# Product with the values in unsplit fp32 on two column groups, one key tile a step, loops written out

## What is computed

```python
# attention: batch 2, 8 heads, 768 tokens, head size 64
q_bucket, k_bucket = ...                 # 6 sign bits of q @ proj and k @ proj
scores = scale * np.matmul(q, k.transpose(0, 1, 3, 2))
scores = np.where(q_bucket == k_bucket, scores, -1000000000.0)
attn = np.exp(scores - np.max(scores, axis=-1, keepdims=True))
attn = attn / (np.sum(attn, axis=-1, keepdims=True) + 1e-09)
x = np.matmul(attn, v)
# second layer: gate = sigmoid(causal convolution of x, 5 taps), d_model 512
y = gate * (x @ w_val) @ w_out
# third layer: mixes of y with its previous token, d_ff 1024
k = np.maximum(xk @ w_k, 0.0); v = k * k @ w_v
out = sigmoid(xr @ w_r) * v
```

## Time and profile before

| | |
|---|---|
| median of 3 runs | 560.13 us (557.92 to 560.45) |
| span of the profiled execution | 556.6 us |
| its start up to step 0 of the first pair | 22.3 us |
| pair 0, pair 6 (pairs 1 to 5 alike) | 30.5, 31.5 us |
| pair 7 up to the second chunk's convolution | 44.3 us |
| from there to the end | 270.8 us |
| PE busy | 504.8 us, 91% of the span |
| DVE, ACT, POOL busy | 384.0, 327.1, 279.0 us |
| granted TensorE clock, pairs 0 to 6 | 1.00 of 2.4 GHz |

### The profile page before, as it was taken

The page is one execution under the profiler, slowest core; times in us unless marked ns, Lnnn a source line. Parts: engine busy times, 40 slices in busy tenths (PEclk is TensorE's granted clock), DMA queues, the critical chain, the costliest instruction groups (busy, mean ns, idle before and its releaser), DMA issues.

```text
span 556.6 us, 12146 instructions
## 1 busy us (share of the span) xinstructions
PE 504.8 (91%) x3744; PEld 463.4 (83%) x3744; DVE 384.0 (69%) x732; ACT 327.1 (59%) x745; POOL 279.0 (50%) x314
## 2 busy tenths in 40 slices
PE   2699999999999999997895879899799799799997
PEld 0488888878788888875795879899799799799997
DVE  2488887879788787979989778357557638633421
ACT  2398898989899998996744443242251341334140
POOL 4075574747567575757244363462550652544340
PEclk9999999999999999999898989899899899899999
DMA  8958293865839384662100000100100100000101
GB/s 232 217 134 189 98 204 100 204 153 153 206 98 204 113 193 109 140 147 113 39 2 2 0 1 1 39 1 2 38 0 0 38 0 0 20 19 1 39 1 39
DMA packets 20796, 45.74 MB, mean 82 GB/s; under 512 B 3744, under 2 KB 8864, under 8 KB 20768
## 3 DMA queue, kind: packets, MB, share of 16 engines
q1 hardware_dynamic: 20768, 45.38, 32.3%
HBM read 17.06 MB, written 3.15 MB: 36 GB/s over the span
## 4 chain that ended last, share of the span: by engine, by line
PE 62%; DVE 24%; issue 5%; ACT 3%; SPq 2%; DMA 2%; DVEq 1%; POOL 1%; ACTq 0%
PE ps L729 23%; PE ps L690 12%; PE ps L700 12%; PE ps L713 10%; DVE gate L886 10%; DVE tmp_a L984 3%; DVE gate L883 2%; PE ps L669 2%; DVE tmp_b L982 2%; DMA k<-hot_k 2%; DVE tmp_b L987 2%; PE ps L718 2%; DVE pt_lo L863 1%; DVE negmax L855 1%; SPq L245 1%
## 5 line engine op out<-in xcount | busy, mean ns | idle before, releaser
L863 DVE TENSOR_TENSOR pt_lo<-ps,pt_hi 128x384 fp32r<-128x384 f32 x192 | 97.8, 550 | 22.3 <-ACT pt_hi L524 22.0
L855 DVE TENSOR_REDUCE negmax<-ps 128x1 f32<-128x768 f32 x96 | 91.3, 951 | 27.2 <-PE ps L690 27.2
L690 PE MATMUL ps<-k,q 128*128 128x384 f32 x384 | 92.6, 364 | 11.7 <-DMA k<-hot_k 9.2
L516 ACT ACTIVATE probs<-ps,negmax 128x768 f32<-128x768 f32 x96 | 86.2, 898 | 16.8 <-DVE negmax L855 16.2
L700 PE MATMUL ps<-ident,probs 128*128 128x128 f32 x576 | 86.4, 281 | 7.4 <-DVE pt_lo L863 6.7
L700 PEld LDWEIGHTS ps<-ident,probs 128*128 128x128 f32 x576 | 64.9, 141 | 28.7 <-DVE pt_lo L863 13.5
L524 ACT ACTIVATE pt_hi<-ps 128x384 fp32r<-128x384 f32 x192 | 83.9, 488 | 6.7 <-PE ps L700 6.0
L690 PEld LDWEIGHTS ps<-k,q 128*128 128x128 f32 x384 | 64.0, 193 | 25.3 <-issue 11.4
L713 PE MATMUL ps<-pt_hi,vv 128*128 128x256 f32 x288 | 82.2, 315 | 0.0
L713 PE MATMUL ps<-pt_lo,vv 128*128 128x256 f32 x288 | 72.7, 282 | 0.0
L886 DVE SCALAR_TENSOR_TENSOR gate<-x,conv_sb,gate 128x256 f32<-128x256 f32 x96 | 64.2, 668 | 8.3 <-DVE gate L883 0.2
(11 more groups left out here) (93 smaller groups left out, 1257.8 us busy)
## 6 DMA issues: line engine op xcount, KB each, us to landing
k<-k_hi SPq DMA_DIRECT2D x32, 192.0 KB, 3.0
q<-q_hi SPq DMA_DIRECT2D x32, 192.0 KB, 3.7
w_raw<-w SPq DMA_DIRECT2D x8, 640.0 KB, 5.2
raw_q<-qT SPq DMA_DIRECT2D x8, 384.0 KB, 3.0
raw_k<-kT SPq DMA_DIRECT2D x8, 384.0 KB, 3.6
raw_v<-v SPq DMA_DIRECT2D x16, 192.0 KB, 3.9
k<-k_lo SPq DMA_DIRECT2D x16, 192.0 KB, 4.0
q<-q_lo SPq DMA_DIRECT2D x16, 192.0 KB, 4.1
```

What stands on the lines that cost most here:

```text
L516: act.activation(probs[par][:, :], score[par], ACT.Exp, bias=negmax[:, t % TILES:t % TILES + 1], accum_out=sums[:, t % TILES:t % TILES + 1 ...
L690: last = pe.matmul(ps[:, 2 * par + half, 0:HALF], qq[h][:, q], kk[h][:, half * HALF:(half + 1) * HALF], start=first, stop=not first)
L855: dve.tensor_reduce(negmax[:, t % TILES:t % TILES + 1], score[t % 2], AX.XY, ALU.max, negate=True)\
L863: dve.tensor_tensor(pt_lo[g % 2][dst], tbank[u].rearrange("p (k q) -> p k q", q=P), pt_hi[g % 2][dst], ALU.subtract).then_inc(lo_done, 1)
```

## The change

- The product with the values no longer splits anything. `vals` holds the values as loaded, `pt` the transposed probabilities of a whole head, double buffered. ACT copies the first half of each transposed tile (`first_half_up`), DVE the second (`second_half_up`).
- `product(head, kts)`: for one key tile two fp32 matmuls with 64 x 384 out, on column groups 0 to 63 and 64 to 127, one for each half of the queries. Key tile n of the head before is taken in step n of a head (`PV_STEPS`). The last head's product comes as a block at the end.
- The reciprocals are made once a head; POOL widens them (`widen_reciprocals`), three transposes (`spread`, in the fifth step, tt = 4, through bank 4) lay them out like the product, ACT copies them (`reciprocals_up`), and DVE multiplies the product straight from PSUM into `x` (`normalise`). POOL's part in it, the splits of v, `o_parts` and ACT's copies of the product are gone.
- All of `project` is at t = 0, `match` at t = 3 to 6.
- `x` is one stretch of tokens with a halo only at its start; the copies of halos are gone, `save_last` is a plain copy.
- All loops are written out, waits are on constants. `s_v` has one more wait (`relu_done`), `place` waits in front of each DMA for both heads.

```diff
-        tbank = [ps[:, 4 + s, 0:3 * P] for s in range(2)]
-        o_ps = ps[:, 6, 0:GQ]
-        r_ps = ps[:, 6, GQ:2 * GQ]
+        tbank = [ps[:, 4 + s, 0:HALF] for s in range(2)]
+        tbank3 = [t.rearrange("p (k q) -> p k q", q=P) for t in tbank]
...
+R_STEP = 4
+PV_STEPS = {n: (n,) for n in range(KT)}
+
+MATCH_STEPS = (3, 4, 5, 6)
...
+            def spread(head):
...
+                pe.wait_ge(rcpw_done, head + 1)
+                pe.wait_ge(up_done[0], turn_r(head))
+                for j in range(3):
+                    last = pe.transpose(tbank[0][:, j * P:(j + 1) * P], rcp_w[:, j, :, :], ident[:, :])
+                last.then_inc(tr_done[0], 1)
+
+            def product(head, kts):
...
+                h = head % 2
+                if kts[0] == 0:
+                    pe.wait_ge(v_in[h], 16 * (head // 2 + 1))
+                    pe.wait_ge(up_done[0], turns0(head, KT - 1) + 1)
+                    pe.wait_ge(up_done[1], KT * (head + 1))
+                    wait(pe, x_done, 2 * head)
+                for kt in kts:
+                    for n in range(2):
+                        last = pe.matmul(ps[DH * n:DH * (n + 1), 6, 0:HALF], vals[h][:, kt, :],
+                                         pt[h][:, kt, n * HALF:(n + 1) * HALF],
+                                         start=kt == 0, stop=kt == KT - 1, tile_position=(0, DH * n))
+                if kts[-1] == KT - 1:
+                    last.then_inc(pv_done, 1)
...
+            for g in range(PAIRS * TILES):
+                i, t = divmod(g, TILES)
+                head, tt = divmod(g, KT)
+                if g + 2 < PAIRS * TILES:
+                    scores(g + 2)
+                transposes(g)
+                if tt == R_STEP and head:
+                    spread(head - 1)
+                if i < LAST:
+                    if t == 0:
+                        project(i + 1)
+                    if t in MATCH_STEPS:
+                        match(i + 1, MATCH_STEPS.index(t))
+                elif t >= TILES - 2:
+                    pe.wait_ge(xlo_done, 1)
+                    s_val_tile(0, 2 * (t % 2))
+                    s_val_tile(0, 2 * (t % 2) + 1)
+                if tt in PV_STEPS and head:
+                    product(head - 1, PV_STEPS[tt])
+            spread(NHEADS - 1)
+            product(NHEADS - 1, tuple(range(KT)))
...
+            def second_half_up(g):
+                head, tt = divmod(g, KT)
+                if tt == 0:
+                    wait(dve, pv_done, head - 1)
+                dve.wait_ge(tr_done[1], g + 1)
+                dve.tensor_copy(pt[head % 2][:, 3:6, tt * P:(tt + 1) * P], tbank3[1]).then_inc(up_done[1], 1)
...
+            def normalise(head):
+                rows = (LO, HI)[head % 2]
+                dve.wait_ge(pv_done, head + 1)
+                dve.wait_ge(up_done[0], turn_r(head) + 1)
+                for n, part in enumerate((LO, HI)):
+                    dve.tensor_tensor(x[rows, head // 2, HALO + n * HALF:HALO + (n + 1) * HALF],
+                                      ps[part, 6, 0:HALF], r_sb[part, :], ALU.mult).then_inc(x_done, 1)
...
+                if tt == 0 and head:
+                    add_eps(head - 1)
+                if g + 2 < PAIRS * TILES:
+                    tile_max(g + 2)
+                if tt == 0 and head:
+                    reciprocals(head - 1)
+                second_half_up(g)
+                if tt == 0 and head >= 2:
+                    normalise(head - 2)
...
-                dve.tensor_scalar(z[:, :, 0:1], z[:, :, GQ:GQ + 1], carry[:, bass.ds(c + 1, 1)], None, ALU.mult)\
-                    .then_inc(hist_done, 1)
+                if (c + 1) % CPB:
+                    dve.tensor_copy(z[:, :, 0:1], z[:, :, GQ:GQ + 1]).then_inc(hist_done, 1)
+                else:
+                    dve.memset(z[:, :, 0:1], 0.0).then_inc(hist_done, 1)
```

More of the change, by code:

```diff
@@ L47, with wait, turns0, turn_r @@
 W2_PIECE = W2 // W2_PIECES
[L50 to L56, removed]
+R_STEP = 4
+PV_STEPS = {n: (n,) for n in range(KT)}
+MATCH_STEPS = (3, 4, 5, 6)
+PLACED = 8 * 16
+def wait(eng, sem, count):
+    if count > 0:
+        eng.wait_ge(sem, count)
+def turns0(head, tt):
+    return KT * head + tt + max(0, head - 1) + (1 if head >= 1 and tt > R_STEP else 0)
+def turn_r(head):
+    if head == NHEADS - 1:
+        return turns0(NHEADS, 0)
+    return turns0(head + 1, R_STEP) + 1
 def build(nc, qT, kT, v, proj, w1, w2, conv, mu_k, mu_r, codes, out):
@@ L361, in normalise @@
-            def normalise(i, j, g):
-                h, n = divmod(g, GROUPS // 2)
-                rows = (LO, HI)[h]
-                pool.wait_ge(o_up, j * GROUPS + g + 1)
-                own(i)
-                settled()
-                part = [o_parts[rows, n % 2, k, :] for k in range(3)]
-                step(i, pool.tensor_tensor(part[0], part[0], part[1], ALU.add))
-                own(i)
-                step(i, pool.tensor_tensor(x[rows, j // 4 * CPB + n, j % 4, HALO:XW], part[0], part[2], ALU.mult))
-                own(i)
-                pool.sem_inc(x_done, 1)
@@ L447, in _ @@
-            pairs(pool, body)
+                               base=0, pattern=[[-1, P]], channel_multiplier=1).then_inc(ident_up, 1)
+            low_parts(0)
+            for i in range(PAIRS):
+                if i:
+                    widen_reciprocals(2 * i - 1)
+                if i < LAST:
+                    low_parts(i + 1)
+                split_w(i)
+                if i == LAST:
+                    x_low(0)
+                widen_reciprocals(2 * i)
+            widen_reciprocals(NHEADS - 1)
@@ L618, in s_r @@
             def s_r(c):
-                after(act, o_done, c, DT, 0)
+                wait(act, o_done, c * DT)
                 for m in range(DT):
@@ L636, in _ @@
             tanh_gate(1)
-            def chunk(c, nxt, pre):
+            for c in range(CHUNKS):
                 act.wait_ge(mixlo_done, (c + 1) * 2 * DT)
-                if nxt:
+                if c + 1 < CHUNKS:
                     s_val(c + 1)
-                    if isinstance(c, int) and c == 0:
+                    if c == 0:
                         w2_high((2, 3))
@@ L778, in _ @@
-            pairs(pe, body)
-            output(PAIRS - 1, GROUPS - 1, 0)
-            output(PAIRS - 1, GROUPS - 1, 1)
+            for g in range(PAIRS * TILES):
+                i, t = divmod(g, TILES)
+                head, tt = divmod(g, KT)
+                if g + 2 < PAIRS * TILES:
+                    scores(g + 2)
+                transposes(g)
+                if tt == R_STEP and head:
+                    spread(head - 1)
+                if i < LAST:
+                    if t == 0:
[8 more added lines that the diff above has]
+                    product(head - 1, PV_STEPS[tt])
@@ L831, in chunk @@
                 s_v(c)
-            chunks(pe, chunk)
         @block.vector
@@ L858, in low_parts @@
[L858 to L864 removed]
+                    wait(dve, placed[B], PLACED * p)
@@ L959, in gated @@
+            add_eps(NHEADS - 1)
+            dve.wait_ge(pv_done, NHEADS - 1)
+            reciprocals(NHEADS - 1)
+            normalise(NHEADS - 2)
             def gated(c, m):
```

642 lines of the change are left out of this document (230 added, 412 removed).

## The result

The changed kernel takes **574.62 us** (median of 4 runs, 572.84 to 578.94) against 559.80 (4 runs, 557.92 to 560.45): ratio 1.027 [1.022, 1.032]. The direction was forecast, the size was not: +1.2% had been forecast (567 us), +2.7% came. The profiled execution is the slowest of the four: 578.94 us with a span of 577.1.

A forecast was written before the change was run, and what follows sets the result against it. PE was taken to bound the pairs, DVE the end of attention. Terms 17.5 - 3.2 + 4.3 - 12.0 = +6.6 on the 556.6 span gave 563.2; with 3.5 around it, 567 us, range 546 to 590.

The forecast's parts named there:

- The new wait: First product matmul of heads 2 to 15 waits some 2 us for DVE's `normalise`, 14 times; step 4.62 us.
- the rival without the wait: DVE is ahead, so the wait for `x_done` isn't felt: -27, 540 us; chance 0.07.
- The excursion: PE's move into column groups for one key tile: 0.97 us, 0.70 data and 0.27 going in and out.
- the switch is hidden: Rival: going in and out of column mode costs nothing behind the transposes, -24, 543 us; chance 0.15.
- the groups don't overlap: Rival: column groups of 64 run one after the other, +0.69 on 96 key tiles, +66, 633 us; chance 0.04.
- The clock: Rival: granted clock falls after each new wait, 14 x 1.5 = +21, 588 us; chance 0.10.
- Pairs 1 to 6: Attention's middle pairs: 34.4 us each against 31.47, +2.9 a pair, +17.5 together.
- the two steps with `spread`: Fifth step of each head: three transposes 0.33 and about 0.35 waiting for ACT's copy, 0.68 more.
- The tail: Second chunk's taps to the end: three chunks -6.9, clock falls gone -4.5, halos outside -0.6, together -12.0.
- Pair 0: First pair: six steps without product 12.5 us, second six 14.8; 27.3 against 30.5, -3.2.
- Pair 7: Last pair and block, up to the second chunk's taps: 48.7 against 44.3 us, +4.3, bounds 0 and +9.
- The start: Stretch up to step 0 of pair 0: 22.3 us, no change forecast.

The follow-up runs named there:

- the kernel in threes: Changed kernel with normalise first, spread behind the product, high parts a step later, key tiles in threes instead of one a step: 538.38 us, ratio 0.958.
- the grouped kernel: Changed kernel with normalise first, key tiles taken in twos in steps 1, 3 and 5 of a head: 544.74 us, ratio 0.972.
- the second profile: The changed kernel run again without any edit, beside the experiments: 572.60 us, ratio 1.0245.
- the 538.62: Changed kernel with normalise first, spread behind the product, high parts of the next pair's keys and queries made at t = 2: 538.62 us, ratio 0.960.

## Why the prediction was right in direction and wrong in size

- **The new wait: right, with its mechanism.** Forecast: 14 waits, steps of 4.62 us at t = 0 and 6. Measured: 14 waits, 24.3 us, steps of 4.49 and 4.61. (The working's 2.05 + 0.15 + 0.50 + 1.02 + 0.1 makes 3.82, not 3.85.) Moving `normalise` forward gives 27 us, where the rival without the wait had been priced at 27. That the two are the same number is luck: 23.4 us of waiting went, and with it the clock's two falls of 1.6, which that rival didn't hold. What I didn't draw from my own count was the obvious one: DVE stands idle just before the maximum, and that is where the work belonged.
- **The excursion: right.** Forecast 0.97 for a key tile with 0.27 for going in and out; measured 0.98 and 0.27 to 0.32, with the kernel in threes giving less (1.1 us of busy time for seven). A regular step was 2.33 forecast, 2.35 to 2.36 measured, and the groups run side by side. The rivals "the switch is hidden" and "the groups don't overlap" are out. The Trainium skill (TensorEngine Tiling, Key Properties) says that a change of mode drains TensorE; the steps of the grouped kernel agree.
- **The clock: the step that failed.** The sum has the pairs at clock 1.00; that the clock falls after the new waits was set aside as a rival with a chance of 0.10, on the ground that PE is dense around them, and as all or nothing. It fell after some: in pairs 1, 3 and 6 the step behind t = 6 took 3.8 to 3.9 us for 2.35. These pairs are 36.4 us long for 34.8, together 4.7 us; in the second profile it fell in two, 3.2 us. Pair 3, PE's rows and the granted clock by 1 us:

```profile
146.72 0.87 PE L573 MATMUL ps<-pt,vals 128*64 128x384 f32 x4 [2.03 <-DVE x L721]
147.51 1.09 PE L538 MATMUL ps<-k,q 128*128 128x384 f32 x4
148.40 1.48 PE L549 MATMUL ps<-ident,probs 128*128 128x128 f32 x6
149.81 1.55 PE L573 MATMUL ps<-pt,vals 128*64 128x384 f32 x4
```

```profile
148.00:149.00 1.00, 1.00 (x6) 0.91 (x5) 0.36 (x1) 0.00 (x0) 0.00 (x0) 0.60 0.73 154
149.00:150.00 1.00, 1.00 (x7) 0.67 (x7) 0.68 (x2) 0.51 (x2) 0.00 (x0) 0.50 0.96 283
150.00:151.00 1.00, 1.00 (x4) 0.10 (x2) 0.47 (x1) 0.97 (x2) 0.00 (x0) 0.50 0.96 316
```

  The transposes take 1.48 for 0.81, the product 1.55 for 0.87, and the granted clock is 0.50, 1.2 GHz. I had priced a fall at 1.5; measured 1.6. So the size of one fall was right. What failed is that the sum had none, though the trace of before had shown one behind each wait for `o_out`: an all-or-nothing rival at 0.10, where some of the falls belonged into the sum.
- **Pairs 1 to 6: +17.5 forecast, +24.9 measured.** 4.7 of the difference is the clock. The other 2.6 are 0.4 a pair, in both profiles, and come of a mis-sized term: the two steps with `spread` cost 0.87 more than a regular one where I had 0.68, since the three transposes take 0.52 and not 0.33. Most regular steps are also 0.02 longer than forecast.
- **The tail: -12.0 forecast, -9.7 measured.** I had the clock's fall in the chunks go away three times (-4.5). PE's waits went from 3.1 to 1.5 to 2.6 us, not to under 1, so it went away in some: the chunk from 420.04 has 41.64 us at clock 1.00, the one before it, behind a wait of 2.59, 42.57 at 0.97, and the one after it 43.19 at 0.96. A chunk without a fall was forecast at 40 to 42. In the second profile no chunk has a fall (42.22, 41.42, 41.44) and the tail is -13.2, close to the forecast by two errors against each other: the three chunks give 8.6 where I had 11.4, since DVE still holds PE for 1.3 to 2.7 us, and what lies outside them 4.6 where I had 0.6. (41.4 less 1.5 is 39.9, not the 39.7 of the prediction; PE's busy time in a chunk without a fall is 39.75.)
- **Pair 0: -3.2 forecast, -1.7 measured.** The difference is its first step, 3.88 us where before has 2.29. Its scores and transposes have the lengths of pair 3's slow rows, though the view's clock column has 1.00 there. First the changed kernel, then before:

```profile
25.29 1.62 PE L538 MATMUL ps<-k,q 128*128 128x384 f32 x4 [0.89 <-ACT probs L376]
26.70 1.48 PE L549 MATMUL ps<-ident,probs 128*128 128x128 f32 x6
```

```profile
22.26 0.94 PE L690 MATMUL ps<-k,q 128*128 128x384 f32 x4 [0.88 <-ACT probs L516]
23.04 0.82 PE L700 MATMUL ps<-ident,probs 128*128 128x128 f32 x6
```

  Less these 1.6 us pair 0 is 27.2, and 27.3 was forecast. The written-out kernel with the old product has the same slow rows, the changed kernel that normalises first doesn't: it goes with no edit.
- **Pair 7: +4.3 forecast, +3.9 measured,** a term that was guessed between bounds.
- **The start: 0 forecast, +3.0 measured, and by the other runs no part of the change.** k<-hot_k of the first pair landed 3.0 us later. In the eleven kernels of the experiments the start is 22.0 to 25.3 us long, in the order of nothing that they differ by; the unchanged product with written-out loops has 23.8. Of before there is one profile, so its own spread isn't known.
- **Around the span:** I took 3.5 us, the median of before less the span of its profile. In the runs after, where span and time of the same execution stand side by side, it is 1.8. The profiled execution of before was faster than its median, so my sum had a fast start and a slow frame. That error (1.7 up) hid a little of the others.

In sum: the start +3.0, pair 0 +1.5, pairs +7.4, pair 7 -0.4 and tail +2.3 make, but for rounding, the 13.9 between the spans 563.2 and 577.1. The profiled execution is 4.3 us above the median of its kernel, and the median is 7.6 above the forecast. The clock, in pairs and chunks and at the start of pair 0, is the largest piece. The second profile says the same on a faster execution: of the 6.7 us that its span lies above the forecast 3.2 are the clock in the pairs, 1.6 the first step of pair 0, 2.6 the mis-sized steps and 1.6 the start, less 2.3 in all that pair 0, pair 7 and the tail came out below.

## What to carry to other kernels

A wait is priced by what stands ahead of its release in the queue of the releasing engine; when that engine idles right before, the order of two lines is worth more than the whole rewrite (27 us here, against nothing for the new product itself). Before a change that makes every engine lighter, look at which engine bounds the stretch: DVE, ACT and POOL lost 4 to 11 us a pair, PE 0.6, and the pair could gain no more than PE. And a stretch that gets shorter can meet DMAs that were just in time before: after each step forward, look at which transfer is late next.

## What was not expected of the hardware

- **The clock fell after some waits of one length and not after others.** Of the waits of 2.03 us at t = 6 in pairs 1 to 6 of two profiles of the changed kernel, 5 of 12 were followed by about 3 us at 1.2 GHz; none of the 12 waits of 1.28 us at t = 0 was, nor were single waits of 1.53 and 1.77 in other kernels. In the last pair a wait of 2.41 was followed by a fall in both profiles, one of 2.06 in neither; among the chunks of the first profile one wait of 1.89 was and one wasn't. At 1.6 us each, this is a good part of the 7.2 us between the two spans. What decides it stays open.
- **Unsplit fp32 is no faster than what it replaced.** A key tile in column groups costs 0.65 us beyond the first (2.09 for three, 1.44 for two, 0.80 for one). Six of them, 3.9 us for a head, take the place of six half groups at 0.71 to 0.77, 4.4 us; without excursions that would have been a small gain. With six it is 5.8 us and a loss of 1.4 a head. What went with the old product gives it back: the wait for `pt_lo` (0.36) and the transposes of the reciprocals (0.22) in every second step, 1.7 a head, of which `spread` takes 0.87.
- **The same 192 KB copy took from 4 to 9 us to land.** k<-hot_k has a median of 4.1 us from issue to landing, and the first one 6.0 before and 9.3 after, with the same list of transfers issued ahead of it. It is this spread, not the mean, that decides whether a pair is 30.6 or 32.4 us long. Count the time from SP's first issue in `place` to the turn of the cast to `k_hi`: with 13.9 us and more (the changed kernel twice, and the 538.62) none of 18 pairs was late; with 12.0 to 12.6 us the number of late pairs out of six was 1, 6, 4, 6 and 0 in five kernels, and not in the order of their margins.
